# A delta-rule attention's first chunk pair: inverse and solve taken chunk by chunk, with part of VectorE's work handed to GpSimd

## The reference, cut to what matters

```python
for t in range(S):
    y[:, :, t] = einsum('bhd,bhde->bhe', q[:, :, t], state)
    v_old = einsum('bhde,bhd->bhe', state, kt)        # kt: normalised k
    state = state + bt * einsum('bhd,bhe->bhde', kt, vt - v_old)
```

## Time and profile before

| | |
|---|---|
| time, median of 3 runs (lowest to highest) | 1044.85 us (1043.45 to 1045.12) |
| the profiled execution: its own time, and its span | 1045.29 us, 1043.5 us |
| mean granted TensorE clock | 0.980 |
| busy: TensorE, VectorE, ScalarE, GpSimd | 96%, 69%, 46%, 21% |
| first pair of chunks, to the second part of the first product | 0 to 76.49 us |
| first token tile | 76.5 to 161.8 us |
| second token tile, to its inverse products | 161.8 to 171 us |
| TensorE busy in 76.49 to 98.99 us | 19.63 of 22.50 us |

### The profile page before, as it was taken

How to read it: one execution, slowest core, us unless ns; L and a number is a source line. 1 busy time by engine, 2 the same in 40 slices (tenths; PEclk the granted TensorE clock), 3 DMA queues, 4 the chain that set the end, 5 groups by cost and what they waited for, 6 DMA issues and landing times.

```text
span 1043.5 us, 25843 instructions
## 1 busy us (share of the span) xinstructions
PE 1004.7 (96%) x10445; PEld 934.1 (90%) x10445; DVE 723.3 (69%) x1655; ACT 475.9 (46%) x708; POOL 214.7 (21%) x244
## 2 busy tenths in 40 slices
PE   7888998999999999999999999999999999999994
PEld 7877797889889889889899999999999999999994
DVE  6987545587577578543559776777677686776774
ACT  3622325324423523423254555556465465655553
POOL 0080083030021021031306212112211112212111
PEclk8899998999999999999999999999999999999998
DMA  9340140150160051116646536225252526535221
GB/s 331 91 110 2 37 109 2 56 151 2 42 158 9 17 129 24 28 62 221 199 154 205 161 63 181 49 45 161 45 160 46 167 39 173 167 68 146 42 35 23
DMA packets 71459, 102.04 MB, mean 98 GB/s; under 512 B 28624, under 2 KB 59856, under 8 KB 70992
## 3 DMA queue, kind: packets, MB, share of 16 engines
q1 hardware_dynamic: 59296, 78.51, 24.7%
q0 software_dynamic: 10992, 20.70, 10.4%
q10 hardware_dynamic: 1088, 1.65, 0.5%
HBM read 140.53 MB, written 29.51 MB: 163 GB/s over the span
## 4 chain that ended last, share of the span: by engine, by line
PE 83%; DVE 8%; ACT 3%; POOL 3%; issue 2%; POOLq 0%; DVEq 0%; ACTq 0%
PE ps L1641 40%; PE ps L1805 19%; PE ps L1689 6%; PE ps L1520 3%; PE ps L1816 2%; PE ps L1503 2%; PE ps L1705 2%; PE ps L1620 2%; DVE prod L1010 2%; DVE x L1014 2%; PE ps L1600 2%; POOL x L642 1%; PE ps L1610 1%; POOL pool_prod L639 1%; PE ps L1561 1%
## 5 line engine op out<-in xcount | busy, mean ns | idle before, releaser
L1641 PE MATMUL ps<-xr,wr_in 128*128 128x512 f32 x972 | 241.4, 402 | 1.1 <-DVE h L1104 0.5
L1641 PEld LDWEIGHTS ps<-xr,wr_in 128*128 128x128 f32 x972 | 181.4, 191 | 42.6 <-DVE wr_in L1097 0.9
L1641 PE MATMUL ps<-xbT,w1r 128*128 128x256 f32 x1728 | 211.6, 283 | 0.7
L1641 PEld LDWEIGHTS ps<-xbT,w1r 128*128 128x128 f32 x1728 | 209.7, 192 | 2.5 <-issue 2.5
L1805 PE MATMUL ps<-w2r,hbT 128*128 128x384 f32 x1152 | 205.9, 336 | 0.0
L1805 PEld LDWEIGHTS ps<-w2r,hbT 128*128 128x128 f32 x1152 | 198.9, 188 | 0.0
L670 POOL DMA_INDIRECT out_rows<-yb,idx x55 | 90.2, 1640 | 379.0 <-DVE yb L1322 289.6
L1134 DVE TENSOR_TENSOR w1r<-w1s,w1r 128x768 fp32r<-128x768 f32 x128 | 121.2, 957 | 18.7 <-ACT w1r L807 16.5
L823 ACT ACTIVATE hbT<-ps 128x512 fp32r<-128x512 f32 x96 | 57.4, 598 | 166.6 <-PE ps L1641 166.6
L807 ACT CAST w1r<-w1s 128x768 fp32r<-128x768 f32 x128 | 104.5, 828 | 24.3 <-DMA w1s<-in_we 24.3
L1134 DVE TENSOR_TENSOR w2r<-w2s,w2r 128x768 fp32r<-128x768 f32 x128 | 113.8, 951 | 1.8 <-ACT w2r L811 1.8
(11 more groups left out here) (216 smaller groups left out, 1139.4 us busy)
## 6 DMA issues: line engine op xcount, KB each, us to landing
w1s<-in_we SPq DMA_DIRECT2D x32, 1536.0 KB
w2s<-in_we SPq DMA_DIRECT2D x32, 1536.0 KB
xb<-rows SPq DMA_DIRECT2D x25, 402.0 KB, 3.9
kv_s<-in_kv SPq DMA_DIRECT2D x24, 384.0 KB, 3.5
k_s<-in_k SPq DMA_DIRECT2D x12, 512.0 KB, 3.8
joint<-in_q SPq DMA_DIRECT2D x24, 256.0 KB, 4.7
out_rows<-padrow SPq DMA_DIRECT2D x13, 384.0 KB, 4.3
w_in<-in_w_blocks SPq DMA_DIRECT2D x3, 1152.0 KB, 11.0
```

The costliest lines, as they stand in the source:

```text
L1641: mm = pe.matmul(dst, w, m, start=(opens and n == 0), stop=(closes and n == len(todo) - 1))
```

## The change

- The first pair's low product, corner product, their copies and the solve diagonals are made for chunk 0 first and then for chunk 1, in two sets of banks (`first_low`, `first_corner`, `first_solve`); `solve_u(0)` waits for chunk 0's corner alone. `first_k_q` stands before the base steps' end; ScalarE copies the scores and GpSimd masks them. The off-diagonal blocks of the second pair are copied early to a place in `w_oT` and moved to `off` by GpSimd.
- GpSimd makes the low parts of all the weights (18 operations of 384 elements and one of 2400) and the first pair's `scaled_v`. It no longer makes base steps of the second pair; VectorE makes all 31, the first 12 before the first product. For the third pair GpSimd makes 20 in place of 24.
- The diagonal copies of chunk 1 are split between ScalarE and VectorE; k's columns are loaded in two halves without the padding rows; the norms take one operation less; the first state is copied, half on ScalarE and half on VectorE, and not added.
- 14 warm-up matmuls in place of 8 at the start, spread over banks. Fewer `keep_warm` behind.
- Low, corner and so on move two places later in the first two tiles; in the first tile the gram of chunk 4 stands at the same place as the corner. `rows_of` and the two halves of `norms` for the third pair are placed differently.

```diff
-        POOL_STEPS = {1: 16, 2: 24}
+        POOL_STEPS = {2: 20}
+        FIRST_STEPS = 12
...
-        START = {0: 8, 1: 1}
+        START = {0: 10, 1: 3}
...
-            tight = {"low": 1, "corner": 2, "gram0": 3, "gram1": 4, "k0": 5, "u0": 6, "s0": 7, "k1": 8, "u1": 9,
-                     "s1": 10}
+            tight = {"low": 1, "corner": 2, "gram0": 2, "gram1": 3, "k0": 4, "u0": 5, "s0": 6, "k1": 7, "u1": 8,
+                     "s1": 9}
...
 # GpSimd, before its loop over tiles
+            pool.wait_ge(s_half, 10)
+            pool.wait_ge(s_base, STEPS)
+            scaled_v(0)
+            first_pT()
+            zero_x(1)
+            pool.wait_ge(p_low, 1)
+            pool.wait_ge(s_off, 4)
+            nc.gpsimd.tensor_copy(off[:], off_early).then_inc(s_off_moved, 1)
+            weights_low(0)
+            scaled_v(1)
+            for f in range(1, FT):
+                weights_low(f)
+            pool.wait_ge(s_woh, 1)
+            nc.gpsimd.tensor_tensor(wr_o[:, 1], w_o[:], wr_o[:, 0].bitcast(F32), ALU.subtract).then_inc(s_wo, 1)
...
 # ScalarE
             diagonals_of(0)
-            diagonals_of(1)
+            half_diagonals()
             off_diagonals_of(0)
+            act.wait_ge(s_half_diag, 2)
             off_diagonals_of(1)
             roots(0)
             diagonals_of(2)
             diagonals_of(3)
+            early_off_diagonals_of(2)
+            early_off_diagonals_of(3)
             weights_high()
+            first_k_q()
             out_weights_high()
-            low_times_inverse(0)
-            solve_diagonals(0)
-            corner(0)
-            off_diagonals_of(3)
-            off_diagonals_of(2)
+            first_low(0)
+            first_solve(0, 0)
+            first_low(1)
+            first_solve(0, 1)
+            first_corner(0)
             roots(1)
+            first_solve(1, 0)
+            first_solve(1, 1)
+            first_corner(1)
             u_out(0)
+            first_state()
             y_out(0)
...
 # VectorE
+            half_diagonals()
             rows_of(0)
             norms(0)
+            norm_columns(0)
             base(0, 0, Q - 1)
             columns_of(0)
-            norm_columns(0)
-            scaled_v(0)
             rows_of(1)
-            corner_half()
-            pT_out(0)
-            norms(1)
-            weights_low(0)
-            state_out(0)
-            weights_low(1)
-            scaled_v(1)
+            first_corner_half(0)
+            first_corner_half(1)
+            norms(1, (0,))
+            u_half(0)
+            norms(1, (1,))
+            first_state()
+            base(1, 0, 5)
             r_out(1)
             pT_out(1)
             u_half(1)
             norm_columns(1)
-            weights_low(2)
-            state_out(1)
+            base(1, 5, 10)
             y_half(1)
-            weights_low(3)
+            base(1, 10, FIRST_STEPS)
             x_low(0)
...
 # in the loop over tiles
-                    if t == 0 and n == 0 and f + 4 < FT:
-                        weights_low(f + 4)
-                    if t == 0 and i == PRODUCTS - 6:
-                        split(wr_o[:, 0], wr_o[:, 1], w_o[:], s_woh, 1, s_wo)
+                    if t == 0 and i == place(t, "low"):
+                        state_out(1)
...
 # TensorE
-            keep_warm(D_BANKS, 8)
+            for n in range(14):
+                pe.matmul(ps[:, C_BANKS + n % 4, n // 4 % 2 * P:n // 4 % 2 * P + P], ones[:], ones[:], start=True, stop=True)
...
             fold()
+            first_k_q()
             for k in range(18, Q - 2):
                 keep_warm(E_BANKS + 1, 2, k)
             keep_warm(E_BANKS + 1, 8, Q - 2)
-            low_times_inverse(0)
-            keep_warm(C_BANKS, 4)
-            corner(0)
-            first_k_q()
+            first_low(0)
+            first_low(1)
+            first_corner(0)
+            first_corner(1)
             solve_u(0)
-            keep_warm(E_BANKS, 6)
+            keep_warm(E_BANKS, 4)
             state_step(0)
```

More of the change, by code:

```diff
@@ new lines, in first_k_q, with first_low @@
+            def first_k_q():
+                act.wait_ge(p_rp, 1)
+                for h_ in range(2):
+                    k_q = both_banks(H_BANKS, L)[tokens(h_)].rearrange("p g (a t) -> p (g a) t", t=L)
+                    nc.scalar.copy(q_pT(0, h_, tokens(h_)), k_q).then_inc(s_kq, 1)
+            def first_low(n):
+                act.wait_ge(p_low if n else p_low_first, 1)
+                nc.scalar.copy(first_blocks(low_inv[0], n).rearrange("p (k a) g i -> p k a (g i)", k=2),
+                               ps[:, first_banks(n):first_banks(n) + 2, 0:HP * Q].rearrange("p k (a t) -> p k a t", t=L)
+                               ).then_inc(s_low if n else s_low_first, 1)
@@ L721, in corner @@
                 act.wait_ge(s_solve, cp + 1)
-                for h_ in range(2 if cp else 1):
+                for h_ in range(2):
                     rows = slice(h_ * L, h_ * L + Q)
@@ L1050, in pT_out, with half_diagonals @@
-                last.then_inc(s_pT, 1)
-            def corner_half():
-                dve.wait_ge(p_corner, 1)
-                dve.wait_ge(s_solve, 1)
+                    mask = after_row[rows].unsqueeze(1).unsqueeze(1).to_broadcast([L, 4, PAIRS // 4, L])
+                    last = nc.vector.tensor_tensor(by_four(q_pT(c, h_, rows)), k_products(rows)[:, :, :, D:], mask, ALU.mult)
+                last.then_inc(s_pT, 1)
+            def half_diagonals():
+                cols = slice(PAIRS, 2 * PAIRS)
+                gram = both_banks(gram_banks(1), L).rearrange("p g (a t) -> p g a t", t=L)
+                dve.wait_ge(p_gram, 2)
+                for g in range(2):
+                    rows = slice(L + g * Q, L + g * Q + Q)
+                    nc.vector.tensor_copy(by_bank_pair(diag[rows, cols]), gram[rows, :, :, g * Q:g * Q + Q]
+                                          ).then_inc(s_half_diag, 1)
@@ L1412, in _ @@
                         if i == place(t, "k0"):
+                            if t == 0:
+                                rows_of(cp + 1)
                             r_out(c)
                             pT_out(c)
-                            if cp + 1 < CP:
+                            if t and cp + 1 < CP:
                                 rows_of(cp + 1)
                         if i == place(t, "u0") and cp + 1 < CP:
-                            norms(cp + 1)
+                            norms(cp + 1, (0,) if t == 0 else (0, 1))
+                        if i == place(t, "s0") and t == 0:
+                            norms(cp + 1, (1,))
                         if i == place(t, "s0"):
@@ L1575, in to_xT @@
             def to_xT(cp, n):
-                first = (C_BANKS, D_BANKS)[n]
+                first = x_banks(cp, n)
                 pe.wait_ge(s_y, 4 * cp + 4)
-                if n == 0:
+                if n == 0 and cp:
                     pe.wait_ge(s_state, 2 * cp + 3)
```

247 lines of the change are left out of this document (169 added, 78 removed).

## The result

The changed kernel takes **1062.21 us** (median, 1060.42 to 1063.12) where the kernel before took 1044.96 beside it: a ratio of **1.0166 [1.0149, 1.0184]**, 17.3 us slower. I had said 1037.8, faster, and the time lies outside my range. The profiled execution's span is 1060.1 us, for 1043.5 before, at a mean granted clock of 0.965, for 0.980.

A forecast was written before the change was run, and what follows sets the result against it. It took TensorE as the bound from the third token tile on, so only the first 200 us could move. Arrival -3.7, first tile -0.85 and second -2.7 summed to -7.25, giving 1037.8 us; range 1031 to 1047.

The forecast's parts named there:

- Opening: Start through grams and diagonal copies: more warm-up delays the first gram, cheaper copies give some back; +1.35 us.
- Chunk by chunk: End of the base steps to solve_u(0): chunk 0 going first takes 6.8 us for 9.75; -2.95.
- Solve to state: solve_u(0) to the state step: 3.6 us for 3.9, plus 0.8 for norms running beside GpSimd; +0.5 us.
- State to k-state: State step to k-state: the first state is copied, not added, 3.75 us for 6.0; -2.25.
- k-state itself: The k-state matmuls run at the full clock level, 3.28 us for 4.95; -1.65.
- Contention: VectorE's small operations beside GpSimd's low parts take 1.7 times as long: 4.1 us in the first gap.
- Base steps in the gaps, +0.25: VectorE's first five second-pair base steps, between first state and r, take 4.1 us for 3.85 free; +0.25.
- My rival by that rule: Before the first product: VectorE operations wait for whole GpSimd operations, two per 0.95 us; 1047.3 us, chance 0.20.
- arrival: Start of the first product's second part, at 76.49 us before; forecast 3.7 us sooner, near 72.8.
- k-state to the arrival: k-state to the first product's second part: y and x_low wait less, contention gives back 2.15 and 0.9; +1.05 us.
- First tile: First token tile: TensorE's waits and lower-clock losses fall from 6.15 to 5.3 us; -0.85.
- Second tile: Second token tile up to its inverse products: waits and clock losses fall from 6.4 to 3.7 us; -2.7.

The follow-up runs named there:

- e1: The changed kernel with GpSimd's weight low parts replaced by memsets that write and read nothing, the low parts left out: 1044.91 us, 0.9953 of before.
- f3: e2 with VectorE's base steps placed one place sooner in all tiles but the first: 0.9974 of before.
- f4: e2 with six keep_warm matmuls between the second low product and the first corner product: 0.9973 of before.
- e3: The changed kernel with only w_out's low part (2400 elements) back on VectorE, in the first tile: 1.0099 of before.
- e4: The changed kernel with VectorE's first 12 base steps of the second pair moved behind x's low part: 1.0034 of before.
- g3: The changed kernel with each of GpSimd's 18 low-part operations cut into two of 192 elements: 1.0107 of before.
- e2: The changed kernel with the exchange undone: low parts and scaled_v(1) on VectorE, the second pair's first 12 base steps on GpSimd: 1050.18 us, 0.9995 of before.
- f1: e2 with the first tile's low and corner products one place sooner, so a product stands before gram(4): 0.9971 of before.
- g2: g1 with fewer keep_warm before the first low product: 1041.13 us, 0.991 of before.
- f2: e2 with 8 warm-up matmuls at the start in place of 14: 1.0003 of before.
- g1: e2 with the edits of f1, f2, f3 and f4 together: 1044.29 us, 0.9939 of before.

## Why the prediction was wrong

In the order of its steps, with the starts of the profiled executions.

- **Opening, +1.35: right here, in part by luck.** The gram starts at 6.96 (7.0 said), the base steps end 1.2 us later than before. But the 28 warm-up instructions took 4.75 to 6.28 us in the traces of kernels with this same opening. In e1 and f3 the gram starts at 5.74 and 5.78 and the transpose behind the base steps at 37.45 and 37.50, as before the change. I took the pace of one trace as fixed.
- **Chunk by chunk, -2.95: too much.** `solve_u(0)` starts at 47.34, not 45.5; from the end of the base steps it is 8.7 us for 9.75, so -1.0. TensorE waits 1.19 inside the corner product, and the clock falls to 1.2 GHz there. I had costed TensorE's work at full level in a stretch where the new order itself makes it stand still. f4 shows it: with filler there the clock stays at 2.4 GHz, and the way from the low product to k-state is 1.5 to 2.1 us shorter.
- **Solve to state, +0.5: +1.7.** Again the clock, and filler: the solve took 3.65 (2.07 at full level), and behind it eight filler instructions took 2.07 us at the lower level. The copies of u had ended at 52.0, the filler ended at 53.0, and the state step starts at 52.92.
- **State to k-state, -2.25: -1.85.** Nearly right. With the steps above, k-state starts at the same time as before, where I had it 3.35 us sooner.
- **k-state itself, -1.65: right,** 3.28.
- **Contention ("Base steps in the gaps, +0.25"): the step that failed.** I took the ratio 1.7 from VectorE's long operations beside GpSimd's of like length, and made 4.1 us of the first five steps, 0.25 more than the gap. It was 20.3. A ratio was the wrong form: the cost is a whole GpSimd operation per VectorE operation, whatever the latter's own time. For operations of like size both forms give about the same number, which is why my row could not tell them apart. But the trace of before had a row that could, with the engines exchanged: a GpSimd operation of 87 elements, 0.34 us in its neighbours, that took 3.42 while VectorE ran four two-input operations (last section). No ratio of 1.7 makes that. The Trainium skill (SBUF — State Buffer, Who interferes with whom) had it right: two-input VectorE operations and reading GpSimd operations exclude each other for the whole instruction; e1, e3, e4 and g3 agree (0.2 us per operation beside memsets, 0.585 beside 192 elements, 0.95 beside 384, and one of 31 elements held for 3.93 us). My rival by that rule was too mild as well: it let two VectorE operations through per turn, without any row for that (8.6 us, arrival at 82.7), and let the 2400-element operation fall on the second five steps. One per turn gives 14 operations up to 69.07, two more to 71, and the long turn to 76.4. I gave it 0.20; its direction was right, and its size, +2.0 in all, was an eighth of the 16.5 by which the profiled executions differ. Its time, 1047.3, lay just outside my own range.
- **k-state to the arrival, +1.05: +18.** Of it 15.9 is the wait for `solve_u(1)`, which belongs to the step above; 3.0 is the lower clock behind 16 us of standing still (solve 3.65 for 2.07, its filler 1.65 for 0.94, state step 2.71 for 1.64); and some 0.9 came back, where 2.0 was said for y and x's low part. The second part of the product starts near 92.8: the arrival is 16.3 us later than before, where I had -3.7. Base steps 5 to 12 cost nothing: GpSimd was through by then, at 76.2. I had added 2.15 and 0.9 for them, and the 0.9 doesn't even follow from my own figures, 1.5 us by 1.7 in a gap of 2.5.
- **First tile, -0.85: -0.96,** and by its parts nearly so: inverse 0.67 (0.4 said), corner 2.25 (2.5 said), u wait gone, two drops of the clock.
- **Second tile, -2.7: +1.25.** I assumed that a later low product means a shorter wait. But the base steps of VectorE are tied to places, and two more places of room moved them along: VectorE stood idle 3.09 us before 182.13 and then finished 3.9 late. f3, the same steps one place sooner, takes 1.8 off that wait.
- **Forecast in sum.** -7.25 said, +16.6 in the spans. Of the 24 us between, 17 to 18 are the exchange (e2 against the changed kernel). Even without the turns I would have been wrong: e2 is at 0.9995. The parts in which I saw gain are worth having only with the edits of f1, f3 and f4, and of g2 for the opening.

Not tried: the exchange alone in the kernel before, and the changed opening without the chunk-by-chunk order. How much each adds to e2's zero is therefore open.

## What to carry to other kernels

Before work is moved to GpSimd, list VectorE's two-input SBUF operations that will run beside it: each can cost one whole GpSimd operation, as it did for nearly all 18 here. So what harms is a long GpSimd operation beside many short VectorE ones on the path; cut the GpSimd operation small, or let those steps follow it. When a producer gets faster and the time stays, look at what stands before the consumer in its own queue: filler that keeps the clock up is work too, and less of it was worth about 3 us here. A step that is moved later does not gain slack if the work it waits for is tied to the same places.

## What the runs showed of the hardware that was not expected

GpSimd lost nothing in these turns: 0.955 us per operation with VectorE queueing at each, and 2.90 for three before. With the roles exchanged it is the other way round, and worse. In e2 VectorE ran six low parts and a two-input product without a gap, and GpSimd's 60-element operation (0.3 us in its neighbours) ended only when VectorE paused. VectorE first, then GpSimd:

```profile
56.39 1.48 DVE L1225 TENSOR_TENSOR wr_in<-w_in,wr_in 128x384 fp32r<-128x384 f32 x3
57.79 0.94 DVE L1155 TENSOR_TENSOR kv_s<-kv_s,nrm_t 128x768 f32<-128x768 f32 x1
58.66 1.48 DVE L1225 TENSOR_TENSOR wr_in<-w_in,wr_in 128x384 fp32r<-128x384 f32 x3
```

```profile
55.63 4.67 POOL L694 TENSOR_TENSOR x<-x,pool_prod 128x60 f32<-128x60 f32 x1
```

GpSimd got none of VectorE's seven gaps, where VectorE gets each of GpSimd's. It is no single case: f1, f2, f3 and g1 have such a row of 4.46 to 4.71 us, f4 and g2 one of 2.34, where VectorE pauses after three operations. And so had the kernel before: my prediction says that its trace has no small VectorE operation beside a large GpSimd one, but it had the reverse. VectorE first, then GpSimd:

```profile
56.72 1.48 DVE L1097 TENSOR_TENSOR wr_in<-w_in,wr_in 128x384 fp32r<-128x384 f32 x3
58.12 0.94 DVE L1029 TENSOR_TENSOR kv_s<-kv_s,nrm_t 128x768 f32<-128x768 f32 x1
```

```profile
55.85 3.42 POOL L642 TENSOR_TENSOR x<-x,pool_prod 128x87 f32<-128x87 f32 x1
```

VectorE loses nothing in it (0.49 us per low part). One thing does not fit yet: in all these rows GpSimd's operation starts 0.55 to 0.87 us before VectorE's first low part, beside an operation that reads PSUM, which is time enough to end. Why it didn't, and why VectorE's queue gives no turn there but does in its run of six at 65.09 in e2 (4.94 us, 0.82 each), was not tested.
